# Attention matmuls of blocks 1 to 7 as eight tiles of 64 rows by 32 columns, even and odd heads in a bank each

## What is computed

```python
def phi(x):
    a = np.einsum('rd,bhsd->bhsr', S1, x)
    b = np.einsum('rd,bhsd->bhsr', S2, x)
    return np.einsum('bhsi,bhsj->bhsij', a, b).reshape(*x.shape[:-1], r * r)
q_p, k_p = (phi(q), phi(k))
kv = np.einsum('bhsf,bhsd->bhfd', k_p, v)
z = np.sum(k_p, axis=2)
num = np.einsum('bhsf,bhfd->bhsd', q_p, kv)
den = np.einsum('bhsf,bhf->bhs', q_p, z)[..., None] + 1e-06
return num / den
```

```python
xn = x / sqrt(mean(x * x) + 1e-06) * rms_g
x = silu(xn @ w_gate) * (xn @ w_val) @ w_out       # 128 -> 1536 -> 128
logits = x @ phi                                   # 32 slots
slot_input = softmax over tokens(logits).T @ x     # then per expert relu(. @ w1) @ w2
out = softmax over slots(logits) @ slot_out
```

## Time and profile before

| | |
|---|---|
| median of 3 runs | 295.54 us (294.04 to 296.53) |
| the profiled execution, its own time | 296.13 us |
| its span, first to last instruction | 294.3 us |
| PE busy | 280.9 us (95%) |
| PEld busy | 231.3 us (79%) |
| DVE busy | 230.2 us (78%) |
| ACT busy | 157.1 us (53%) |

### The profile page before, as it was taken

How to read it: one execution, slowest core, us unless ns; L and a number is a source line. 1 busy time by engine, 2 the same in 40 slices (tenths; PEclk the granted TensorE clock), 3 DMA queues, 4 the chain that set the end, 5 groups by cost and what they waited for, 6 DMA issues and landing times.

```text
span 294.3 us, 6608 instructions
## 1 busy us (share of the span) xinstructions
PE 280.9 (95%) x2544; PEld 231.3 (79%) x2544; DVE 230.2 (78%) x443; ACT 157.1 (53%) x302; POOL 33.6 (11%) x58
## 2 busy tenths in 40 slices
PE   6889998999999999999999999999999999999990
PEld 6777876888887888888878878888788878997570
DVE  4778699957999889679988896797689688784532
ACT  2576654634666465446674653465546546556431
POOL 2279110000100100013001000100010003000000
PEclk9999999999999999999999999999999999999995
DMA  6999670227222102212221022179210322410016
GB/s 174 352 219 218 132 218 0 38 36 210 78 35 47 26 7 40 40 28 76 40 42 25 7 44 37 25 266 351 40 27 16 51 33 61 111 25 3 0 54 253
DMA packets 65393, 25.62 MB, mean 87 GB/s; under 512 B 50001, under 2 KB 62034, under 8 KB 65362
## 3 DMA queue, kind: packets, MB, share of 16 engines
q1 hardware_dynamic: 64786, 24.78, 35.4%
q10 hardware_dynamic: 576, 0.43, 0.5%
HBM read 17.45 MB, written 2.23 MB: 67 GB/s over the span
## 4 chain that ended last, share of the span: by engine, by line
PE 79%; SPq 9%; DVE 5%; DMA 2%; issue 2%; ACT 1%; DVEq 0%
PE bank L1112 77%; SPq L389 5%; DMA q_in<-in_q 2%; PE bank L1196 1%; DVE hid L943 1%; DVE area L1104 1%; SPq L395 1%; SPq L413 1%; DVE hl L954 1%; SPq L417 1%; SPq L393 1%; DVE area L829 0%; PE bank L1422 0%; ACT silu L644 0%; PE bank L1209 0%
## 5 line engine op out<-in xcount | busy, mean ns | idle before, releaser
L644 ACT ACTIVATE silu<-bank 128x512 f32<-128x512 f32 (+1 forms) x108 | 61.9, 574 | 78.7 <-PE bank L1112 77.5
L943 DVE TENSOR_TENSOR hid<-bank,silu 128x512 f32<-128x512 f32 (+1 forms) x108 | 70.7, 655 | 27.0 <-PE bank L1112 23.1
L954 DVE TENSOR_TENSOR hl<-hid,hh 128x512 fp32r<-128x512 f32 (+1 forms) x108 | 71.5, 662 | 0.1
L652 ACT ACTIVATE hh<-hid 128x512 fp32r<-128x512 f32 (+1 forms) x107 | 64.5, 603 | 4.2 <-DVE hid L943 3.8
L1112 PE MATMUL bank<-xh,wgh 128*128 128x512 f32 (+1 forms) x109 | 42.6, 391 | 0.2 <-DVE hid L943 0.2
L1112 PE MATMUL bank<-hh,woh 128*128 128x512 f32 (+1 forms) x108 | 42.5, 394 | 0.2 <-DVE hl L954 0.2
L1112 PE MATMUL bank<-xh,wgl 128*128 128x512 f32 (+1 forms) x109 | 41.2, 378 | 0.0
L1112 PE MATMUL bank<-hh,wol 128*128 128x512 f32 (+1 forms) x108 | 41.1, 380 | 0.0
L1112 PE MATMUL bank<-xh,wvl 128*128 128x512 f32 (+1 forms) x108 | 41.1, 380 | 0.0
L1112 PE MATMUL bank<-xh,wvh 128*128 128x512 f32 (+1 forms) x109 | 41.1, 377 | 0.0
L1112 PE MATMUL bank<-hl,woh 128*128 128x512 f32 (+1 forms) x108 | 41.0, 380 | 0.0
(11 more groups left out here) (158 smaller groups left out, 333.6 us busy)
## 6 DMA issues: line engine op xcount, KB each, us to landing
area<-in_moe_w SPq DMA_DIRECT2D x8, 512.0 KB, 5.5
area<-in_moe_w SPq DMA_DIRECT2D x1, 4096.0 KB, 12.8
area<-area SPq DMA_DIRECT2D x112, 32.0 KB, 2.0
q_in<-in_q SPq DMA_DIRECT2D x16, 128.0 KB, 3.4
y_nat<-in_v SPq DMA_DIRECT2D x4, 512.0 KB, 7.9
out<-area SPq DMA_DIRECT2D x8, 256.0 KB, 3.0
area<-in_k SPq DMA_DIRECT2D x14, 128.0 KB, 6.7
y_nat<-area SPq DMA_DIRECT2D x112, 16.0 KB, 1.8
```

What stands on the lines that cost most here:

```text
L644: act.activation(silu[n][:, 0:w], gate_b[n][:, 0:w], ACT.Silu).then_inc(s_silu_ready, 1)
L652: act.activation(hh[m % NH][:, 0:w], hid[m % 2][:, 0:w], ACT.Copy).then_inc(s_hh_ready, 1)
L943: dve.tensor_tensor(hid[n][:, 0:w], val_b[n][:, 0:w], silu[n][:, 0:w], ALU.mult).then_inc(s_hid_ready, 1)
L954: dve.tensor_tensor(hl[m % NH][:, 0:w], hid[m % 2][:, 0:w], hh[m % NH][:, 0:w].bitcast(F32), ALU.subtract).then_inc(s_hl_ready, 1)
```

## The change

In blocks 1 to 7 each attention matmul now takes one head and 32 tokens: 64 rows (the head's features), 32 stationary columns (tokens) and 33 moving columns (its moments alone, without the zeros). That is 2 head pairs by 4 token tiles by 4 groups of 32 tokens by 2 heads, 64 matmuls (128 records) in place of 16 (32 records). The even heads go to `bank_a`, the odd to `bank_b`. DVE's instructions stay as many and as long; the two that write `x_at` now write every second group of 32 columns each. Block 1 waits for both halves of its features ahead of the whole burst and not between its halves. Blocks 0 and 8 are as before.

```diff
+        def by_parity(jn):
+
+            return 0 < jn < NB
+
...
+                x_v = x_at[:, :, :].rearrange("p t (h d) -> p (t h) d", h=H)
+                x_y = x_at[:, :, :].rearrange("p t (g y d) -> p (t g) y d", y=2, d=D)
...
-                    x_v = x_at[:, :, :].rearrange("p t (h d) -> p (t h) d", h=H)
-                    ins = dve.tensor_tensor(x_v[:, i * n:(i + 1) * n, :], nd[:, :, 0:D],
+                    ins = dve.tensor_tensor(x_y[:, :, i, :] if by_parity(jn) else x_v[:, i * n:(i + 1) * n, :], nd[:, :, 0:D],
                                             rden[:, i * n:(i + 1) * n].unsqueeze(2).to_broadcast([P, n, D]), ALU.mult)
...
+                if by_parity(jn):
+                    if jn < NF:
+                        pe.wait_ge(s_qpT_ready, HP * jn + HP - 1)
+
+                    for hp in range(HP):
+                        for t in range(HT):
+                            for x in range(P // NS):
+                                rows, tok = slice(x * NS, (x + 1) * NS), slice(t * P + x * NS, t * P + (x + 1) * NS)
+                                for y, bk in ((0, bank_a), (1, bank_b)):
+                                    f, c0 = slice(y * FT, (y + 1) * FT), (t * HP + hp) * DA
+                                    ins = mm(bk[rows, c0:c0 + DA], qpT[jn % 2][f, hp, tok], kv[f, b, hp, y * DA:(y + 1) * DA])
+                    ins.then_inc(s_nd_ps, 1)
+                    return
                 for hp in range(HP):
...
-                    if 0 < jn < NF and hp == 1:
-                        pe.wait_ge(s_qpT_ready, HP * jn + HP - 1)
```

## The result

The changed kernel takes 300.29 us (median of 4 runs, 299.06 to 303.73) beside 295.84 for the kernel before on the same chip (median of 4, 294.04 to 296.53): ratio 1.0143, interval 1.0097 to 1.019. It is 4.5 us slower, more than the 1% that I set as the bound to no change, though the lower end of the interval touches that bound. The profiled execution took 300.27 us.

The account below looks back on a forecast made before the run. PE was taken to bound the kernel from 46 us on. Six blocks at 1.07 + 0.13 - 0.98 = +0.22 us add 1.3 to the 295.54 us median, giving 296.8 us, range 293.6 to 303.5.

Parts of the forecast that it names:

- likeliest case: Whole kernel: time stays within 1% (3 us) of the kernel before; given 69%.
- the one on instructions: PE's program: 1344 more instructions, five more fetches, taken as nothing; upper end one 1.2 us fetch per block, 7 us.
- The burst, 127 x 8.4 = 1.07 us: Attention in blocks 2 to 7: 128 records at the pace of logits, replacing 32 records of 0.98 us.
- The second change of shape: Between the attention burst and `s_blk`: a new gap as tile shape changes, 0.13 us a block.
- +0.22 a block: Blocks 2 to 7: sum of 1.07 + 0.13 - 0.98 us each, +1.3 us for six.
- Block 1 hidden: Block 1's longer burst costs nothing, as PE has 1.00 us free in that stage; without that cover +0.2.
- The stationary columns alone set a tile's pace: All bursts: a tile takes 58 ns for 64 stationary columns, 34 for 32; halving the moving columns changes nothing.
- a long burst runs out of supply: Attention burst: instructions arrive too slowly, records at 10.6 to 27 ns; 303.4 us at 17 ns, 311.0 at 27; 20%.
- The last sign: Whole kernel: a time above 300 with a 1.3 us burst would mean a cost somewhere not looked at.
- Eight tiles divide by eight: Attention burst: all eight tiles overlap, 4.2 ns a record, -0.32 us a block, 293.6 us in all; 7%.
- Strips and halves don't multiply: Attention burst: only the two row halves overlap and strips follow in turn, 17 ns a record, 303.4 us; 9%.
- The rule that I weighed: Attention burst: about 60 cycles of overhead per matmul, so 25 ns a record, +2.3 us a block, 309.6 us in all.

Follow-up runs that it names:

- run 8: Kernel before, with attention in blocks 2 to 7 as 128 rows by 32 stationary by 66 moving columns and projections as 32 by 64; 294.92 us, ratio 0.997.
- run 10: Changed kernel with its 64 matmuls over all 128 rows and the loops turned so that four column strips take turns; 299.85 us, ratio 1.0111 to the kernel before.
- run 4: Changed kernel with 64 tokens a matmul: row halves kept, half the instructions, 64 records a burst; 297.17 us, ratio 1.0034 to the kernel before.
- run 1: Changed kernel with its 64 matmuls over all 128 rows, no row halves, two matmuls in a row per strip; 301.15 us, ratio 1.0178 to the kernel before.

## Why the prediction was right in part and wrong in its likeliest case

**The step that failed** is the one on instructions: "Five more are to be expected, some within a burst. No burst of today uses 256 instructions in a microsecond. I take nothing". The five fetches came (25 on the page), and two of all fetches cost 2.6 us on PE's path. I had costed a fetch at 1.2 us from the page's share and kept 7 us as an upper end, so it lay in the range (300.3 within 293.6 to 303.5) but not in the sum. The argument for nothing was that the longest burst of before, of 256 instructions too, runs evenly. It does so at 27 ns a record, 3.7 us in all, longer than the 2.3 to 2.7 us from a fetch's start to its use; the changed burst takes 1.1. That the time lies in the range is partly luck: its upper end was reckoned from rivals with a pace of 17 ns, which didn't come.

With that the likeliest case, "same" at 69%, was wrong: the kernel is slower by 1.4%, with only the interval's lower end, 1.0097, inside the 1% of that case. Without the two stops, 2.6 us by the trace, it would by this estimate have stayed within that 1%. Point by point:

- **PE bounds from 46 us on, each us of PE is a us of the kernel.** Right: behind block 1 the shift of every later instruction grows by what PE loses (0.13 us ahead of block 2, 0.41 behind its burst, 5.66 at the end) and none of it is recovered.
- **The burst, 127 x 8.4 = 1.07 us.** Right: 1.10 at 8.65 ns.
- **The second change of shape, 0.13 us.** Right: 0.12.
- **+0.22 a block.** 0.28 measured: 0.03 from the pace, and `s_blk` to `hh` takes 0.61 and not 0.57 us. +1.7 for +1.3.
- **Block 1 hidden.** Right: DVE takes its result 0.13 us later, and was that late before, from a transfer of `q_in`.
- **The stationary columns alone set a tile's pace.** Right for 64 of them, where 66 and 33 moving columns go at the same pace. Wrong for 32: run 8 shows 59 ns of a tile with 66 moving columns, the changed kernel and run 10 far less with 33. The sum didn't need it, for it took the pace of logits.
- **DVE at nothing.** Right: its products take 411 to 426 ns, median 423.
- **What I hadn't listed:** the short gaps beside SP's transfers of tokens, 1.1 us in four blocks. No row of before could show them: its bursts have 64 instructions in 0.93 us, and run evenly.

Of the rivals, *a long burst runs out of supply* is the one that came nearest, with 20%, but in another form. I had it as a slower pace, 10.6 ns and more through the burst; what came was the pace of logits, held to the end, and a stop for the fetch that the sentence on what would show it names. The last sign came true as well: a time above 300 with a burst of 1.3 us (1.29) meant a cost that I had not looked at. *Eight tiles divide by eight* falls for a burst of this length (8.65 ns and not 4.2), though its first 32 records do come at 6. *Strips and halves don't multiply* falls by run 4. The rule that I weighed, from the Trainium skill, page "TensorEngine Tiling (Array Packing)", section "Instruction Overhead", would have given 25 ns a record; 128 records in a row at 8.65 contradict it as a floor for records in different tiles.

## What to carry to other kernels

Cutting a matmul into more tiles multiplies instructions, and the first pace that it meets may be that of the instructions and not of the array: count them, and compare the time in which a burst uses a fetch's worth with the time from a fetch's start to its use. A fetch that costs nothing in slow stretches costs its whole lateness in a fast one, and shows in front of an instruction that the change never touched; move the count by some filler and see whether the wait moves with it. If halving the moving columns saved nothing at this number of stationary columns, those zeros were free there, and the instructions that remove them are not.

## What the hardware showed that I had not expected

- Records of small tiles start every 8.2 ns in the long run, 4.1 ns an instruction, and the first 32 of a burst behind long matmuls every 6 ns, with a pause of 0.09 us between. At half the granted clock the burst's records came at 10.3 ns in place of 8.65, those of logits at 13.4 in place of 8.4.
- PE stopped for instructions, 0.55 to 1.66 us from start to start, at places 56 short of a multiple of 256, in or just behind bursts that use 256 instructions in little over 1 us, and went on 2.3 to 2.7 us after a fetch of 16 KB had begun.
- Bursts of 256 instructions show gaps of up to 178 ns while SP's transfers of tokens go on, and none beside its transfers of weights; bursts of 128 at 14.5 ns a record show none.
- With 32 stationary columns the moving ones count: 14.8 ns a record for 66 in four tiles, 8.7 for 33; with 64 stationary columns 66 and 33 go alike (30 and 29 ns in two tiles).
- Two matmuls that follow each other in the same strip cost pace even at this rate: 10.1 against 8.7 ns a record by the order of the loops alone (runs 1 and 10).
